# First chunk's products with u moved to GpSimd, loads reordered, and VectorE's bonus sum placed before the mask of its own step

## The chip, the cores and the metric

One core of one Trainium2 chip runs the whole program. The metric is the device time in microseconds of one execution, the median of several runs.

## The reference

Three layers in float32. First a linear attention over 4 batches, 8 heads, 768 tokens and 48 channels per head; its output, laid out as 3072 tokens of 384 numbers, goes through a soft mixture of experts (8 experts, 4 slots each) and then through a dense layer of width 2048 with a sigmoid gate. The change touches only the first layer:

```python
state = np.zeros((B, H, D, D), dtype=np.float32)
for t in range(S):
    kt, vt, rt = (k[:, :, t], v[:, :, t], r[:, :, t])
    cur = np.einsum('bhd,bhe->bhde', u[None] * kt, vt)
    y[:, :, t] = np.einsum('bhd,bhde->bhe', rt, state + cur)
    state = w[None, :, :, None] * state + np.einsum('bhd,bhe->bhde', kt, vt)
...
logits = x @ phi        # softmax over tokens and over slots, 8 experts: relu(slot @ w1) @ w2
...
h = x @ w_in
return (h * (1.0 / (1.0 + np.exp(-1.702 * h)))) @ w_out
```

The term with `u` is the "bonus": for each token and head, the sum over the 48 channels of r times k times u, times the token's v.

## The kernel before

The 768 tokens are cut into 6 chunks of 128, and in each chunk the 4 batches are done one after the other: 24 steps, numbered n = 4c + b for chunk c and batch b. Chunk 0 is written out, chunks 1 to 4 are a hardware loop, and chunk 5 is written out again. While the steps run, the weights of the expert layers are loaded beside the inputs of the steps. After step 23 come the expert layers and then the dense layer, in which TensorE does most of the work; nothing of that part is changed.

The order of the work is written out by hand for each engine, and semaphores tie the engines together. What one step consists of:

- **SyncE's queue** issues the loads of step n: `rk` (r and k with the channels on the partitions, 512 KB, tile `rkb`, two buffers), `kr` (k and r with the tokens on the partitions, 384 KB, tile `krb`, two buffers) and `v` (192 KB), and from chunk 1 on one or two 512 KB pieces of expert weights. The load of `rk` for step n waits until VectorE has scaled step n-2, and the load of `kr` for step n waits until GpSimd has made `kk` of step n-2.
- **VectorE** in step n: `scale` of step n+1 (L772, two operations, writes `rks`), which waits for the load and for `earlier` of step n-1 on TensorE (the last reader of the buffer); `mask` of step n (L798, two operations, copies the causal part of the scores into `at`); `bonus_sum` of step n+1 (L786, writes `dds`); `new_state` of step n-1 (L807). In a batch with b = 1 `slot_max` of the chunk before stands ahead of these, and with b = 3 `running` stands before `new_state`.
- **GpSimd** in step n: `bonus` (L1204, r times k into `rkn`, then L1209, times u, but in chunk 0 only the first of the two: there VectorE does the second at L782), `scaled_keys` (L1216, `kk`), `bonus_values` (L1226, writes `vd` from v and `dds`, so it waits for `bonus_sum` of step n). In the last chunk there are no `scaled_keys`; after the step with b = 1 eight small operations build `own` (L1245, L1246), after b = 2 the row maxima are subtracted (L1251), and in b = 3 the row factors are multiplied (L1240) before `bonus_values`.
- **TensorE** in step n: `earlier` of step n-1 (L414), `scores` of step n (L378), `outputs` of n-1 (L426), `state` of n-1 (L438), `tokens` of n-2 (L447), and from chunk 1 on, at the end of the step, `bonus_turns` of step n itself (L397), which reads `vd` of step n. In chunk 0 `bonus_turns` of the step before stands ahead of `outputs` instead, but for the last step of the chunk, which has both. `scores` wait for the masks of the step before and for `scale` of their own step.

Each engine takes its instructions in the order written, so an engine that waits holds all that stands behind the wait. In this text e is the time at which TensorE begins `earlier` in a step.

## Time and profile before

| | before |
|---|---|
| median of 3 runs | 385.12 us (384.98 to 385.4) |
| the profiled execution | 385.27 us, of which 383.5 us lie between its first and last instruction |
| TensorE busy | 369.9 us (96%), granted clock 1.00 throughout |
| VectorE, ScalarE, GpSimd busy | 235.0, 189.4, 94.5 us |
| data moved | 63.76 MB, nearly all in the first 160 us |

Busy time counts an engine's instructions, not its waits; for TensorE the ends of matmuls are modelled, so its share is high even where it is held up a little. The share is a mean over the whole span. What a change to the first layer is worth is read from the first 130 us: from the start of each instruction, and from what ended the idle time before it.

### The profile page before, as it was taken

To read this page: it belongs to the slowest core of one execution; us is meant where nothing else is said; L and a number is where in the kernel's file an instruction comes from. 1 tells how busy PE (TensorE), PEld (TensorE's weight loads), DVE (VectorE), ACT (ScalarE), POOL (GpSimd) and SP (SyncE) were. 2 spreads that over 40 slices of the span, in tenths; PEclk is the share of its full clock that TensorE was granted. 3 is DMA by queue.
4 is the path that set the end of the run, shared out by engine and by line. 5 is a ranking of instruction groups with operands and counts; after the bars stand their busy time and mean duration, and the time that the engine had idled before them with its cause. 6 is when DMAs were issued, how large, how long until landed. Compare 5 with 4: busy or idle time off the path is not lost.

```text
span 383.5 us, 9099 instructions
## 1 busy us (share of the span) xinstructions
PE 369.9 (96%) x3206; PEld 290.6 (76%) x3206; DVE 235.0 (61%) x433; ACT 189.4 (49%) x409; POOL 94.5 (25%) x110
## 2 busy tenths in 40 slices
PE   5698999999999999999999999999999999999996
PEld 5677788878777344577888888888888888888885
DVE  6978787878774301587756556555555555555550
ACT  1344554545434440676564456445644564465452
POOL 4678788878682020100000000000000000000000
PEclk9999999999999999999999999999999999999999
DMA  7899999999999999600011002000200020002002
GB/s 234 286 333 344 400 393 405 399 393 354 405 327 409 390 414 413 249 0 2 1 46 38 0 0 84 0 0 0 82 0 0 0 82 0 0 0 82 0 2 82
DMA packets 21797, 63.76 MB, mean 166 GB/s; under 512 B 3088, under 2 KB 6816, under 8 KB 21392
## 3 DMA queue, kind: packets, MB, share of 16 engines
q1 hardware_dynamic: 20864, 63.09, 43.4%
q10 hardware_dynamic: 912, 0.39, 0.5%
q8 instruction: 14, 0.23, 0.2%
q14 instruction: 7, 0.06, 0.0%
HBM read 58.75 MB, written 4.72 MB: 165 GB/s over the span
## 4 chain that ended last, share of the span: by engine, by line
PE 92%; DVE 2%; DMA 2%; issue 1%; ACT 1%; POOL 1%; SPq 0%; DVEq 0%; ACTq 0%
PE bank L638 11%; PE bank L637 11%; PE bank L636 11%; PE bank L378 6%; PE pair L426 6%; PE pair L636 6%; PE pair L637 6%; PE pair L638 6%; PE bank L623 4%; PE pair L414 3%; PE pair L397 3%; PE bank L585 3%; PE bank L447 3%; PE bank L565 2%; DMA vb<-v 2%; PE bank L438 2%
## 5 line engine op out<-in xcount | busy, mean ns | idle before, releaser
L926 DVE TENSOR_TENSOR gf<-bank,sg 128x512 f32<-128x512 f32 x72 | 49.8, 691 | 58.3 <-ACT sg L1133 58.0
L1133 ACT ACTIVATE sg<-bank 128x512 f32<-128x512 f32 x72 | 42.9, 598 | 71.0 <-PE bank L623 71.0
L637 PE MATMUL bank<-ghi,whi 128*128 128x512 f32 x190 | 73.9, 389 | 0.0
L636 PE MATMUL bank<-glo,whi 128*128 128x512 f32 x190 | 73.9, 389 | 0.0
L638 PE MATMUL bank<-ghi,wlo 128*128 128x512 f32 x190 | 73.9, 389 | 0.0
L937 DVE TENSOR_TENSOR glo<-gf,ghi 128x512 fp32r<-128x512 f32 x96 | 66.3, 691 | 0.3
L1139 ACT ACTIVATE ghi<-gf 128x512 fp32r<-128x512 f32 x95 | 59.3, 624 | 1.8 <-DVE gf L926 1.7
L636 PEld LDWEIGHTS bank<-glo,whi 128*128 128x128 f32 x190 | 35.7, 188 | 7.4
L637 PEld LDWEIGHTS bank<-ghi,whi 128*128 128x128 f32 x190 | 35.7, 188 | 7.4
L638 PEld LDWEIGHTS bank<-ghi,wlo 128*128 128x128 f32 x190 | 35.7, 188 | 7.4
L772 DVE TENSOR_TENSOR rks<-rkb,bank 112x512 f32<-112x512 f32 x48 | 30.8, 681 | 15.4 <-PE pair L414 10.9
L636 PE MATMUL pair<-glo,whi 128*128 128x512 f32 x95 | 37.3, 392 | 0.0
L637 PE MATMUL pair<-ghi,whi 128*128 128x512 f32 x95 | 37.0, 389 | 0.0
L638 PE MATMUL pair<-ghi,wlo 128*128 128x512 f32 x95 | 37.0, 389 | 0.0
L798 DVE COPY_PREDICATED at<-keep,bank 128x512 f32<-128x512 int32 x48 | 32.5, 730 | 1.3 <-PE bank L378 0.9
L378 PE MATMUL bank<-rks 48*128 48x128 f32 x384 | 27.9, 284 | 5.2 <-DVE rks L772 3.9
L926 DVE TENSOR_TENSOR gf<-pair,sg 128x512 f32<-128x512 f32 x24 | 16.6, 692 | 23.8 <-ACT sg L1133 23.7
L378 PEld LDWEIGHTS bank<-rks 48*128 48x128 f32 x384 | 23.4, 187 | 9.5 <-issue 8.0
L1016 ACT ACTIVATE yt<-pair 112x512 f32<-112x512 f32 x24 | 14.3, 598 | 30.0 <-PE pair L426 30.0
L623 PE MATMUL bank<-ct,mst 128*128 (+1 forms) x72 | 27.9, 392 | 0.5 <-DVE mst L964 0.4
L1204 POOL TENSOR_TENSOR rkn<-krb 128x384 f32<-128x384 f32 x24 | 24.1, 1004 | 12.2 <-DMA krb<-kr 11.9
L426 PE MATMUL pair<-at,vb 128*48 128x128 f32 x384 | 25.9, 277 | 0.0
(179 smaller groups left out, 512.3 us busy)
## 6 DMA issues: line engine op xcount, KB each, us to landing
ring<-w SPq DMA_DIRECT2D x24, 512.0 KB, 6.3
rkb<-rk SPq DMA_DIRECT2D x23, 512.0 KB, 6.2
krb<-kr SPq DMA_DIRECT2D x24, 384.0 KB, 5.5
ring<-w SPq DMA_DIRECT2D x4, 1536.0 KB, 14.3
ring<-w SPq DMA_DIRECT2D x8, 768.0 KB, 8.4
vb<-v SPq DMA_DIRECT2D x24, 192.0 KB, 5.5
out<-ob SPq DMA_DIRECT2D x18, 256.0 KB, 2.1
ring<-win SPq DMA_DIRECT2D x3, 1024.0 KB, 14.3
```

Of the source, the lines that this page charges most:

```text
L378: last = pe.matmul(SC[i][:, hp * CH:(hp + 1) * CH], rks[s, b % 2, 1, hp, :], rks[s, b % 2, 0, hp, :], start=True, stop=True)
L426: last = pe.matmul(YT[i][o0:o0 + D, a * CH:(a + 1) * CH], vb[:, b, 2 * (a + 2 * w) + i, :], at[:, b % 2, i, a + 2 * w, :], start=False, st ...
L623: pe.matmul(HB[f % 4][:, :], mst[:, f * P:(f + 1) * P], ct_flat[:, bass.ds(i * TT, TT)], start=True, stop=True).then_inc(hh_ps, 1)
L636: pe.matmul(o, w_hi, lo, start=(f == 0), stop=False)
L637: pe.matmul(o, w_hi, hi, start=False, stop=False)
L638: pe.matmul(o, w_lo, hi, start=False, stop=(f == KF - 1)).then_inc(prod_ps, 1)
L772: dve.tensor_tensor(rks[a, b % 2, x, :, :], rkb[a, b % 2, x, :, :], w[a, :, :], ALU.mult)\
L798: dve.copy_predicated(at[:, b % 2, half, :, :], keep[:, :].unsqueeze(1).to_broadcast([P, 4, CH]), SC[half][:, :].rearrange("p (h t) -> p h ...
L926: dve.tensor_tensor(gf[:, f % 2, :], bank[f % 4][:, :], sg[:, f % 2, :], ALU.mult).then_inc(gf_ok, 1)
L937: dve.tensor_tensor(glo[:, f % 4, :], gf[:, f % 2, :], ghi[:, f % 4, :], ALU.subtract)\
L1133: act.activation(sg[:, f % 2, :], bank[f % 4][:, :], ACT.Sigmoid, scale=1.702).then_inc(sg_ok, 1)
L1139: act.activation(ghi[:, f % 4, :], gf[:, f % 2, :], ACT.Copy).then_inc(ghi_ok, 1)
```

## The change

Eight edits. (1) In chunk 0 GpSimd multiplies by u itself (L1209 in all chunks) and VectorE's four operations at L782 are gone. (2) The load of u moves from ScalarE's queue to SyncE's, as its fourth load, behind `rk` and `kr` of step 0, with a semaphore of its own. (3) The loads of steps 2 and 3 stand in another order: rk2, v2, rk3, kr2, v3, kr3 in place of rk2, kr2, v2, rk3, kr3, v3. (4) VectorE's `bonus_sum` in step n is that of step n, not n+1, and stands behind `scale` of n+1 and ahead of `mask` of n. (5) In steps 1 to 3 `scale` of the next step stands ahead of `mask`, and in step 0 behind `mask` and `bonus_sum`. (6) ScalarE no longer decays the state in chunk 0, where it is zero, and the counts that VectorE waits for follow. (7) Ten opening matmuls on the identity become nine. (8) Seven such matmuls behind the first scores become six.

```diff
--- before.py
+++ after.py
@@ -40,7 +40,7 @@
 LOWEST = -3.0e38
 EPS = 1e-9
 LEAD = 3
-WARM = 10
+WARM = 9
 
 
 def wait(eng, sem, value):
@@ -190,6 +190,7 @@
             sem(n) for n in ("sc_ps", "masked", "yt_ps", "yt_ok", "st_ps", "sdec", "s_new", "yn_ps", "yn_ok"))
         lt_ps, l_ok, cm_ok, nm_ok, ex_ok, al_ok, tr_ps, tr_ok, p_ps, run_ok = (
             sem(n) for n in ("lt_ps", "l_ok", "cm_ok", "nm_ok", "ex_ok", "al_ok", "tr_ps", "tr_ok", "p_ps", "run_ok"))
+        s_u = sem("s_u")
         nm_new, l_new, mask_go, tiles_go = (sem(n) for n in ("nm_new", "l_new", "mask_go", "tiles_go"))
         spr_ok, bc_ps, nf_ok, fac_ok, lf_ok, ls_ps, samef_ok, rden_ok, si_ps, si_ok = (
             sem(n) for n in ("spr_ok", "bc_ps", "nf_ok", "fac_ok", "lf_ok", "ls_ps", "samef_ok", "rden_ok", "si_ps",
@@ -294,12 +295,17 @@
 
             load_rk(0, 0)
             load_kr(0, 0)
+            sp.dma_start(ubc[:, :, :].rearrange("p h e -> p (h e)"), u.partition_broadcast(P)).then_inc(s_u, 16)
             load_rk(0, 1)
             load_v(0, 0)
             load_kr(0, 1)
             load_v(0, 1)
-            step(0, 2, 0, 0)
-            step(0, 3, 0, 0)
+            load_rk(0, 2)
+            load_v(0, 2)
+            load_rk(0, 3)
+            load_kr(0, 2)
+            load_v(0, 3)
+            load_kr(0, 3)
 
             for dst, src in ((same[:, :], match), (jcol[:, :], jsel), (pick[:, :, :], sel)):
                 sp.dma_start(dst, src).then_inc(s_late, 16)
@@ -384,7 +390,7 @@
                     for i in range(HP):
                         last = pe.transpose(YN[:, i * P:i * P + PAIR], wks[0:PAIR, i, :], idt[0:PAIR, 0:PAIR])
                     last.then_inc(wkn_ps, 1)
-                    keep_warm(LG, 7)
+                    keep_warm(LG, 6)
 
             def bonus_turns(c, b):
 
@@ -774,13 +780,6 @@
 
             def bonus_sum(c, b):
                 n = B * c + b
-                if is_first(c):
-
-                    dve.wait_ge(rk_ok, n + 1)
-                    if b == 0:
-                        dve.wait_ge(s_const, 16 * 2)
-                    dve.tensor_tensor(rkn[:, b % 2, :, :], rkn[:, b % 2, :, :], ubc[:, :, :], ALU.mult)\
-                       .then_inc(rku_ok, 1)
                 dve.wait_ge(rku_ok, n + 1)
                 wait(dve, vd_ok, n - 1)
                 dve.tensor_reduce(dds[:, b % 2, :], rkn[:, b % 2, :, :], AX_X, ALU.add).then_inc(dd_ok, 1)
@@ -789,7 +788,7 @@
                 n = B * c + b
                 if is_first(c, b):
                     dve.wait_ge(zeroed, 5)
-                    dve.wait_ge(s_const, 16 * 2)
+                    dve.wait_ge(s_const, 16)
                 for half in range(2):
                     dve.wait_ge(sc_ps, 2 * n + half + 1)
                     wait(dve, yt_ps, n - 1)
@@ -803,7 +802,11 @@
             def new_state(c, b):
                 n = B * c + b
                 dve.wait_ge(st_ps, n + 1)
-                dve.wait_ge(sdec, HP * (n + 1))
+
+                if is_first(c):
+                    dve.wait_ge(s_new, 1)
+                else:
+                    dve.wait_ge(sdec, HP * (n - B + 2))
                 dve.tensor_tensor(st[a, b, :, :].rearrange("p h e -> p (h e)"),
                                   st[a, b, :, :].rearrange("p h e -> p (h e)"), ST[a, 0:HP * D], ALU.add)\
                    .then_inc(s_new, 1)
@@ -848,17 +851,17 @@
                 more = not (is_last(c) and b == B - 1)
                 if tail and b == 1:
                     slot_max(c - 1)
-                if is_first(c) and b:
+                if is_first(c, b):
                     mask(c, b)
+                    bonus_sum(c, b)
                     scale(*following(c, b))
                 else:
                     if more:
                         scale(*following(c, b))
+                    bonus_sum(c, b)
                     mask(c, b)
                 if is_last(c) and b == 2:
                     row_sum(*early)
-                if more:
-                    bonus_sum(*following(c, b))
                 if tail and b == 3:
                     running(c - 1)
                 if not is_first(c, b) and not is_last(prev(c, b)[0]):
@@ -869,7 +872,6 @@
             scale(0, 0)
             dve.tensor_tensor(wks[a, :, :], wk[a, :, :], pw[a, 7, :].unsqueeze(2).to_broadcast([PAIR, HP, CH]),
                               ALU.mult).then_inc(wks_done, 1)
-            bonus_sum(0, 0)
             steps(dve, step)
 
             def low_weights(which, t):
@@ -993,9 +995,7 @@
         @block.scalar
         def _(act):
             act.dma_start(idt[:, :], ident).then_inc(s_ident, 16)
-            for dst, src in ((ubc[:, :, :].rearrange("p h e -> p (h e)"), u.partition_broadcast(P)),
-                             (keep[:, :], strict)):
-                act.dma_start(dst, src).then_inc(s_const, 16)
+            act.dma_start(keep[:, :], strict).then_inc(s_const, 16)
 
             act.wait_ge(wkn_ps, 1)
             act.activation(wkn[:, :, :].rearrange("p (h i) e -> p h i e", h=HP), YN[:, :].rearrange("p (h i e) -> p h i e", h=HP, i=2)[:, :, :, 0:D],
@@ -1061,7 +1061,7 @@
                     scales(c - 1)
                     kept_logits(c - 1)
                 if not is_first(c, b):
-                    if not is_last(prev(c, b)[0]):
+                    if not is_first(prev(c, b)[0]) and not is_last(prev(c, b)[0]):
                         decay(*prev(c, b))
                     columns(*prev(c, b))
                     if tail and b == 1:
@@ -1203,9 +1203,9 @@
                 wait(pool, dd_ok, n - 1)
                 pool.tensor_tensor(rkn[:, s, :, :], krb[:, s, 0, :, :], krb[:, s, 1, :, :], ALU.mult)\
                     .then_inc(rk_ok, 1)
-                if is_first(c):
-                    return
                 pool.wait_ge(rk_ok, n + 1)
+                if is_first(c, b):
+                    pool.wait_ge(s_u, 16)
                 pool.tensor_tensor(rkn[:, s, :, :], rkn[:, s, :, :], ubc[:, :, :], ALU.mult).then_inc(rku_ok, 1)
 
             def scaled_keys(c, b):
```

VectorE's instructions of chunk 0 before, from behind `wks` to the end of step 1 and the start of step 2 (`rkn` is the product r times k, `dds` the bonus sum, `rks` the scaled r and k, `at` the mask's output, `st` the state):

```order
L782 TENSOR_TENSOR rkn<-rkn,ubc 128x384
L786 TENSOR_REDUCE dds<-rkn 128x8
L772 TENSOR_TENSOR rks<-rkb,bank 112x512 x2
L798 COPY_PREDICATED at<-keep,bank 128x512 x2
L782 TENSOR_TENSOR rkn<-rkn,ubc 128x384
L786 TENSOR_REDUCE dds<-rkn 128x8
L798 COPY_PREDICATED at<-keep,bank 128x512 x2
L772 TENSOR_TENSOR rks<-rkb,bank 112x512 x2
```

The same place of the changed program, where lines have moved by a few (L778 is `scale`, L785 `bonus_sum`, L797 `mask`, L810 `new_state`):

```order
L797 COPY_PREDICATED at<-keep,bank 128x512 x2
L785 TENSOR_REDUCE dds<-rkn 128x8
L778 TENSOR_TENSOR rks<-rkb,bank 112x512 x4
L785 TENSOR_REDUCE dds<-rkn 128x8
L797 COPY_PREDICATED at<-keep,bank 128x512 x2
L810 TENSOR_TENSOR st<-st,bank 112x192
```

The products with u are gone; the first bonus sum now stands behind the first mask; and four scalings, those of steps 1 and 2, stand together.

VectorE's first loop step (b = 0 of a chunk) before:

```order
L772 TENSOR_TENSOR rks<-rkb,bank 112x512 x2
L794 REGISTER_ALU
L49 REGISTER_ALU
L798 COPY_PREDICATED at<-keep,bank 128x512
L794 REGISTER_ALU
L798 COPY_PREDICATED at<-keep,bank 128x512
L784 REGISTER_ALU
L786 TENSOR_REDUCE dds<-rkn 128x8
```

and in the changed program:

```order
L778 TENSOR_TENSOR rks<-rkb,bank 112x512 x2
L783 REGISTER_ALU
L49 REGISTER_ALU
L785 TENSOR_REDUCE dds<-rkn 128x8
L793 REGISTER_ALU
L797 COPY_PREDICATED at<-keep,bank 128x512
L793 REGISTER_ALU
L797 COPY_PREDICATED at<-keep,bank 128x512
```

Within a step the sum has moved ahead of the mask; what the rows do not show is that it is the sum of step n, where before it was that of step n+1, so that counted in steps it comes almost a step later.

GpSimd's first instructions behind its memory sets in the changed program (before, the two rows of L1209 were not there):

```order
L1204 TENSOR_TENSOR rkn<-krb 128x384
L1209 TENSOR_TENSOR rkn<-rkn,ubc 128x384
L1226 TENSOR_TENSOR vd<-vb,dds 128x2x4x48
L1216 TENSOR_TENSOR kk<-krb,wkn 128x384
L1204 TENSOR_TENSOR rkn<-krb 128x384
L1209 TENSOR_TENSOR rkn<-rkn,ubc 128x384
L1216 TENSOR_TENSOR kk<-krb,wkn 128x384
L1226 TENSOR_TENSOR vd<-vb,dds 128x2x4x48
```

From the second step on GpSimd's round in chunk 0 is now the one of all other chunks: two products, `kk`, `vd`.

## Rows read from the trace of the kernel before

**Rows 1.** Waits of TensorE: total us, times, longest us.

```profile
PE bank L378 <- DVE rks L772: 3.9, 3, 1.8
```

**Rows 2.** Timeline of the opening: start us, us, then the instruction.

```profile
2.84 4.05 PE L365 MATMUL bank<-idt 128*128 128x128 f32 x20 [2.84 <-DMA idt<-ident]
...
6.77 1.29 DVE L772 TENSOR_TENSOR rks<-rkb,bank 112x512 f32<-112x512 f32 x2 [1.58 <-DMA rkb<-rk]
...
8.20 1.16 PE L378 MATMUL bank<-rks 48*128 48x128 f32 x16 [1.32 <-DVE rks L772]
9.13 0.56 DVE L782 TENSOR_TENSOR rkn<-rkn,ubc 128x384 f32<-128x384 f32 x1 [0.47 <-POOL rkn L1204]
...
13.06 1.00 POOL L1216 TENSOR_TENSOR kk<-krb,wkn 128x384 f32<-128x384 f32 x1
13.14 1.34 DVE L782 TENSOR_TENSOR rkn<-rkn,ubc 128x384 f32<-128x384 f32 x1 [0.42 <-POOL rkn L1204]
...
26.10 0.65 PE L414 MATMUL pair<-rks,st 48*48 48x128 f32 x16
```

**Rows 3.** Busy times in one stretch; last columns TensorE's clock, DMA share, GB/s.

```profile
2.80:6.90 4.10, 4.05 (x20) 3.86 (x20) 2.52 (x29) 0.66 (x1) 1.32 (x1) 1.00 0.83 229
```

**Rows 4.** Timeline of GpSimd: one `vd` and the next, a full round apart.

```profile
23.06 0.83 POOL L1226 TENSOR_TENSOR vd<-vb,dds 128x384 f32<-128x384 f32 x1 [1.22 <-DVE dds L786]
...
26.86 0.83 POOL L1226 TENSOR_TENSOR vd<-vb,dds 128x384 f32<-128x384 f32 x1
```

**Rows 5.** Timeline of an ordinary step, chunk 4, b = 2.

```profile
92.31 0.65 PE L414 MATMUL pair<-rks,st 48*48 48x128 f32 x16
...
93.10 1.28 DVE L772 TENSOR_TENSOR rks<-rkb,bank 112x512 f32<-112x512 f32 x2 [0.68 <-PE pair L414]
...
94.30 1.36 DVE L798 COPY_PREDICATED at<-keep,bank 128x512 f32<-128x512 int32 x2
...
95.56 0.53 DVE L786 TENSOR_REDUCE dds<-rkn 128x8 f32<-128x384 f32 x1
95.84 0.65 PE L397 MATMUL pair<-idt,vd 128*112 128x128 f32 x4
```

**Rows 6.** Timeline of steps with b = 0, in chunks 4 and 5.

```profile
82.96 0.65 PE L414 MATMUL pair<-rks,st 48*48 48x128 f32 x16
...
84.39 1.28 DVE L772 TENSOR_TENSOR rks<-rkb,bank 112x512 f32<-112x512 f32 x2 [0.23 <-issue]
...
101.30 0.65 PE L414 MATMUL pair<-rks,st 48*48 48x128 f32 x16
...
102.28 1.29 DVE L772 TENSOR_TENSOR rks<-rkb,bank 112x512 f32<-112x512 f32 x2
```

**Rows 7.** Timeline of the last chunk, b = 1 to 3.

```profile
106.11 0.18 POOL L1245 MEMSET own<- 128x96 f32 x1
...
107.17 1.28 DVE L772 TENSOR_TENSOR rks<-rkb,bank 112x512 f32<-112x512 f32 x2 [0.20 <-PE pair L414]
...
107.61 1.01 POOL L1204 TENSOR_TENSOR rkn<-krb 128x384 f32<-128x384 f32 x1
...
108.69 1.01 POOL L1209 TENSOR_TENSOR rkn<-rkn,ubc 128x384 f32<-128x384 f32 x1
...
113.68 0.73 ACT L1055 ACTIVATE lnat<-lnat 128x640 f32<-128x640 f32 x1
113.84 0.65 PE L397 MATMUL pair<-idt,vd 128*112 128x128 f32 x4 [0.17 <-ACT yt L1016]
114.44 0.82 DVE L821 TENSOR_REDUCE rm<-lnat 128x20 f32<-128x640 f32 x1 [0.41 <-ACT lnat L1055]
115.86 1.26 POOL L1240 TENSOR_TENSOR lnat<-lnat,rm 128x640 f32<-128x640 f32 x1 [1.37 <-DVE rm L825]
118.77 0.60 PE L397 MATMUL pair<-idt,vd 128*112 128x128 f32 x4
```

**Rows 8.** The tile `krb`: from a load's issue to its landing.

```profile
DMA to landing us min/median/max: 3.2/5.5/8.4
```

## The prediction

> **What bounds the kernel now.** I read the totals first: TensorE is busy 369.9 of 383.5 us, so time is lost or won where TensorE waits or is made to wait. Its list of waits comes next. The largest that the list shows is 3.9 us for the scaled r and k, three times [rows 1]; with the 2.8 us until the identity has landed [rows 2] it falls into the opening. From 26.10 on TensorE runs from one instruction into the next. So there are two places to look at: the opening, where the change can win, and the 20 steps behind it, where it can only lose.
>
> In the opening TensorE's scores begin when the first `rk` has landed and been scaled: VectorE starts at 6.77, TensorE at 8.20, and `earlier` of the first loop step, the end of the opening for TensorE, starts at 26.10 [rows 2].
>
> An ordinary step shows how tight the rest is [rows 5]. TensorE begins at e = 92.31. VectorE's `scale` starts at e + 0.79, since it waits for `earlier`; its second half ends 1.20 later, where `mask` starts. `bonus_turns`, which reads `vd`, starts at e + 3.53 and waits for nothing, as its `vd` was made a step ahead: the sum that stands at 95.56 is that of the next step.
>
> **The change part by part.** Its own time before is 385.27 us (a span of 383.5 and 1.77 around it); the median of 385.12 lies 0.15 below, so I take 0.15 off at the end.
>
> *Opening.* u is 192 KB, and its load ran beside the first `rk`, in a stretch in which 229 GB/s were moved [rows 3]. 192 KB by that rate is 0.86 us, so with u behind it the first `rk` should land 0.86 earlier and `scale` start at 5.9 in place of 6.77. Scores begin 1.43 behind it, as now, and take 1.16: they end at 8.5. The first mask (1.36 [rows 5], about 0.1 behind the scores) ends at 9.95 and the first sum (0.53) at 10.5, and GpSimd starts `vd` of step 0. Its round then sets the pace: from one `vd` to the next it takes 3.80 with both products in it [rows 4], as it now has in chunk 0. `vd` and `kk` of step 0 take 0.78 and 0.97 to the next start, so the products of step 1 begin at 12.3, those of step 3 two rounds later at 19.9, and `vd` of step 3 starts 3.02 behind them and ends at 23.75. TensorE takes it up 0.1 later, turns it in 0.57, and begins `earlier` at 24.4 in place of 26.10: **-1.7**. VectorE must fit into this round: scale 1.20, sum 0.53 and mask 1.36 are 3.1, with a short state update less than 3.80. Bounds: if the first `rk` lands no earlier, -0.85; if u cost it twice its share, -2.6.
>
> The second product on VectorE took 1.34 where the first took 0.56 [rows 2]: it began beside a `kk` of GpSimd (13.06 to 14.06) and ended 0.42 after it. With the products on GpSimd this wait is gone, which is inside the sum above, since GpSimd's round sets the pace there. The Trainium skill (SBUF — State Buffer, section "SBUF: two separate sides") says that VectorE and GpSimd share one port pair under an exclusive lock: a vector instruction with two SBUF inputs is held for the whole of a GpSimd instruction that reads SBUF. By that rule the trace agrees with 1.34.
>
> u's load, now the third in SyncE's queue, delays the loads behind it by 0.86; GpSimd needs u only for a product at about 7.5, whose sum waits behind a mask until 9.95, so it costs nothing. Cover gone, it would cost its 0.86, as in the lower bound. The order of loads of steps 2 and 3 brings `rk` 3 ahead of `kr` 2; both are asked for (12.3) more than 3 us before GpSimd reads `kr` 2 (16.1), so I take nothing. The decays that are dropped run on ScalarE, which waits for TensorE anyway: nothing. The nine opening matmuls take 0.20 a pass (20 passes in 4.05 [rows 2]) and end at 6.5, before the scores at 7.3: nothing.
>
> *The 19 or so steps behind it.* `vd` of a step is now made within the step. From the start of `scale`: 1.20, sum 0.53, 0.08 to GpSimd, `vd` 0.83, and about 0.1 to TensorE, in all 2.75. In an ordinary step that is e + 0.79 + 2.75 = e + 3.54, and `bonus_turns` is due at e + 3.53 [rows 5]. So most of a step of slack is used up to the last tenth. I take 0.03 for each of 14 such steps, **+0.4**; bounds 0 and 0.1 each, 1.5.
>
> With b = 0 it is later, because VectorE comes out of `running` and `new_state` behind TensorE: `scale` starts at e + 1.43 in chunk 4 (84.39 against 82.96) and at e + 0.98 in chunk 5 (102.28 against 101.30) [rows 6]. The same instructions stand ahead of it in the changed order, only sum and mask have changed places. `vd` is then ready at e + 4.18 and e + 3.73, that is 0.65 and 0.2 late; less 0.05 for what the step before was held, about 0.6 in each of the chunks 2 to 4 and 0.2 in chunk 5: **+2.0**. TensorE has nothing behind to make up for it. Bounds: 0.2 in each of four, 0.8, and 0.75 in each, 3.0.
>
> *Last chunk.* GpSimd has the `own` tiles to build (106.11 to 107.61, 1.50) between `vd` of step b = 1 and the products of b = 2 (107.61 to 109.70, 2.09) [rows 7]. Now `vd` of b = 1 cannot start before 107.17 + 1.20 + 0.53 + 0.08 = 108.98. Then `own` from 109.76, products 111.26 to 113.35, sum to 113.9, `vd` to 114.8, TensorE at 114.9 in place of 113.84: 1.05 late. Behind that `vd` stands the subtraction (1.26, as long as the multiplication at 115.86) to 116.0, the exponential (0.73) to 116.8, row sum to reciprocal (114.44 to 115.86, 1.42) to 118.2, the multiplication to 119.5, `vd` of b = 3 to 120.35, TensorE at 120.45 in place of 118.77: **+1.7** in all. Bounds: the first wait alone, less the 0.17 it covers, 0.9; and 2.2 if the first load of `kr` in it is late too.
>
> Sum: -1.7 + 0.4 + 2.0 + 1.7 = +2.4, 387.65 for a profiled execution, **387.5** as a median.
>
> **The rivals.**
>
> *Faster.* The mechanism is that `vd` comes in time with b = 0 too: `scale` starts at e + 0.8 to 0.98 in all chunks, and in the last chunk only the first wait remains. Then -1.7 + 0 + 0.8 + 0.9 is 0.0, and with an opening of -2.6 it is -0.9: 384.3. For it speaks that chunk 5 shows e + 0.98; against it that the loop's round shows 1.43, and that the turn to the next round lies in it. It decides at the point where all waits of TensorE for `vd` together are less than what the opening gives. 0.17, at 384.3.
>
> *Cancelled.* Opening and waits are of one size, as the 0.0 just worked out: 385.1. 0.12.
>
> *The loads starve.* `vd` of a step now ends at e + 3.44; two products (2.1) and a `kk` (1.0) behind it, at about e + 6.5, `kr` of three steps on from e is asked for, and it is due when GpSimd wants it, 3.1 ahead of its own `vd` at e + 2.6 of that step. That leaves three steps of 4.1 to 4.9 less 6.5 and 0.5, some 6.1 to 7.1 us, where a landing takes 5.5 and at most 8.4 [rows 8]. If landings stay as spread as now, half of the 20 steps could be held by 0.3: +3, 390.5. Against it speaks that requests which come later find a shorter queue. 0.07.
>
> *VectorE is held by GpSimd.* At the chunk's turn VectorE's small two-input operations fall beside GpSimd's products. The hold seen is 0.42 behind the start of a product [rows 2]; if the start of `scale` with b = 0 came later by twice that in each of the three loop rounds, it would be +2.5: 390.0. By the skill's rule named above a hold may last a whole GpSimd instruction, which has the same effect. 0.06.
>
> **How the numbers follow.** Forecast 0.58, faster 0.17, cancelled 0.12, starved 0.07, held 0.06. The likeliest case gives 387.5; its own range, with its terms moved inside their bounds, is 386.1 to 389.3. To hold eight in ten the range goes from 384.5, which leaves out about half of the faster case, to 389.6, which leaves out the two slow rivals: 0.1 and 0.1. About 0.2% (0.77 us) is what a measurement of this kernel can tell from no change. Slower by over that: 0.58 + 0.07 + 0.06 = 0.71; within: 0.12; faster: 0.17.
>
> **What the changed profile would show.** `scale` of step 0 starts near 5.9, and `earlier` of the first loop step near 24.4. The waits of TensorE hold a new line, `bonus_turns` for `vd`, with some 4 us in total: about 0.6 in each b = 0 step of the loop, one of about 1 and one of over 0.5 in the last chunk, near nothing elsewhere. GpSimd in turn waits for `dds` in nearly every step. From the end of the last step on everything stands at one distance to before. I am wrong if the line sums to less than 2 us, or if the opening gives over 3, or if GpSimd waits for `kr` and TensorE behind it.

## The result: 12 us slower, four fifths of it unforeseen

| | before | changed |
|---|---|---|
| median | 385.24 us (383.87 to 387.06, 6 runs) | 397.49 us (395.33 to 400.68, 6 runs) |
| the profiled execution | 385.27, span 383.5 | 398.65, span 396.9 |

The ratio is 1.032 (95% interval 1.027 to 1.037). The forecast of 387.5 (384.5 to 389.6) had the sign right and the size wrong by 10 us.

The page of the changed kernel: the span, TensorE's busy time, and the strips of TensorE's granted clock and of the DMA engines' share, each sign a fortieth of the span.

```profile
span 396.9 us, 9072 instructions
PE 375.5 (95%) x3202; PEld 293.6 (74%) x3202; DVE 234.7 (59%) x429; ACT 186.0 (47%) x397; POOL 97.8 (25%) x114
PEclk9996999999999999999999999999999999999999
DMA  6899889999999979940002000200100020002002
```

Its waits: total us, times, longest us. SPq is SyncE's queue.

```profile
DVE rks L778 <- DMA rkb<-rk: 10.7, 5, 3.1
PE pair L403 <- POOL vd L1226: 9.9, 11, 2.0
POOL rkn L1204 <- DMA krb<-kr: 2.4, 2, 1.9
SPq L278 <- POOL kk L1216: 47.4, 20, 4.0
```

The queue's wait for `kk` in the kernel before, and its wait for VectorE's `scale`, before and then changed:

```profile
SPq L277 <- POOL kk L1216: 27.3, 18, 3.7
SPq L269 <- DVE rks L772: 19.0, 17, 3.9
SPq L270 <- DVE rks L778: 7.5, 5, 4.8
```

The first row of TensorE's wait list before was 3.9 us for the scaled r and k [rows 1]. Now `bonus_turns` (L403) waits 9.9 us for `vd`, where the forecast said some 4. Two other rows were not in the forecast at all: VectorE's `scale` waits 10.7 us for the load of `rk` (3.8 before), and SyncE's queue waits 47.4 us for `kk` before it can ask for `kr`. Part of that wait has only moved: before, the queue stood as long for either, 27.3 us for `kk` and 19.0 for `scale`; now it is 47.4 and 7.5, so that the sum rose from 46.3 to 54.9. GpSimd itself hardly waits for `kr` (2.4 us).

The starts of `earlier` locate the loss. The first is at 25.88 (26.10 before [rows 2]), the last at 132.68 (119.30 before). That difference, 13.4 us, is the whole difference of the spans, so nothing behind the chunks matters. By steps (from one `earlier` to the next, worked out from the timelines; the last row is a run that comes below, e13):

```
chunks 2, 3, 4, 5     b=0                     b=1                     b=2                     b=3
before                5.12 5.11 5.11 5.05     4.24 4.24 4.24 4.03     4.89 4.89 4.89 4.82     4.15 4.20 4.10 4.10
changed               6.03 6.18 6.11 5.82     4.57 4.57 4.57 4.18     4.88 4.89 4.88 5.79     4.95 5.63 5.09 4.96
e13                   6.04 6.14 6.13 5.80     4.57 4.57 4.56 4.18     4.88 4.89 4.89 5.79     4.15 4.15 4.11 4.95
chunk 1: before 5.11 5.85 4.88 4.18; changed 7.39 7.15 4.89 4.27; e13 5.31 4.56 4.89 4.26
```

One figure of the kernel before is not an ordinary step: in the second step of chunk 1 (5.85 where the later chunks take 4.24) TensorE stood for 1.20 us behind the first twelve matmuls of `earlier`, with nothing in the trace that it waited for:

```profile
33.05 0.42 PE L414 MATMUL pair<-rks,st 48*48 48x128 f32 x4 [1.20 <-issue]
```

The same step takes 5.33 to 5.68 in e2, e8, e10 and e12 and 4.24 in e6 and e14, below; no run shows what it is. The changed kernel has no such row.

So of 13.4: opening -0.2; b = 0 +3.75; b = 1 +1.15; the last chunk's b = 2 and 3 +1.8; b = 3 in chunks 2 to 4 +3.2; chunk 1 +3.7.

A step with b = 3 in the changed kernel (chunk 3), which ends at 91.28 with the next `earlier`:

```profile
76.55 1.00 POOL L1216 TENSOR_TENSOR kk<-krb,wkn 128x384 f32<-128x384 f32 x1
77.71 0.33 SPq L278 DMA_DIRECT2D krb<-kr  x1
80.54 0.33 SPq L270 DMA_DIRECT2D rkb<-rk  x1
...
85.65 0.65 PE L420 MATMUL pair<-rks,st 48*48 48x128 f32 x16
...
87.92 1.28 DVE L778 TENSOR_TENSOR rks<-rkb,bank 112x512 f32<-112x512 f32 x2 [3.12 <-DMA rkb<-rk]
89.12 0.55 DVE L785 TENSOR_REDUCE dds<-rkn 128x8 f32<-128x384 f32 x1
89.74 0.83 POOL L1226 TENSOR_TENSOR vd<-vb,dds 128x384 f32<-128x384 f32 x1 [2.53 <-DVE dds L785]
90.63 0.65 PE L403 MATMUL pair<-idt,vd 128*112 128x128 f32 x4 [1.33 <-POOL vd L1226]
```

Read it from the end. TensorE waits for `vd`, `vd` for the sum, and the sum stands on VectorE behind a `scale` that has waited 3.12 us for `rk`. The loads of `rk` around here landed 6.4 to 7.2 us after they were asked for, so the one that ends this wait is that of 80.54. It was asked for so late because it stands in the queue behind `kr` of the step before, two pieces of w (only steps with b = 3 load two) and v; that `kr` had waited for `kk`, which ended at 77.55. And `kk` stands on GpSimd behind `vd`. The circle is closed: a late `vd` makes the next `kk`, `kr` and `rk` late, and with them a later `vd`. It starts at the steps with b = 0, where `vd` is late by the sum's place in the order.

### The profile page after: what moved, and what is told of

Its sections match the earlier page's. It is cut to its first block, busy times and chain, and to the rows that moved or that the text cites. A ratio compares the mean times of both kernels' runs of the same rounds, so it can differ in the third digit from the quotient of the medians.

```text
span 396.9 us, 9072 instructions
## 1 busy us (share of the span) xinstructions
PE 375.5 (95%) x3202; PEld 293.6 (74%) x3202; DVE 234.7 (59%) x429; ACT 186.0 (47%) x397; POOL 97.8 (25%) x114
## 4 chain that ended last, share of the span: by engine, by line
PE 73%; POOL 9%; issue 6%; DMA 5%; DVE 4%; SPq 1%; DVEq 1%; ACT 0%; POOLq 0%; ACTq 0%
PE bank L642 11%; PE bank L643 11%; PE bank L644 11%; PE pair L642 6%; PE pair L643 5%; PE pair L644 5%; PE bank L629 4%; DMA rkb<-rk 3%; PE bank L591 3%; PE bank L384 2%; POOL vd L1226 2%; POOL rkn L1209 2%; POOL rkn L1204 2%; PE bank L571 2%; POOL kk L1216 2%
## 5 line engine op out<-in xcount | busy, mean ns | idle before, releaser
L778 DVE TENSOR_TENSOR rks<-rkb,bank 112x512 f32<-112x512 f32 x48 | 30.8, 682 | 20.8 <-DMA rkb<-rk 10.7
L797 DVE COPY_PREDICATED at<-keep,bank 128x512 f32<-128x512 int32 x48 | 32.2, 725 | 2.5 <-PE bank L384 2.5
L384 PE MATMUL bank<-rks 48*128 48x128 f32 x384 | 29.7, 297 | 3.6 <-DVE at L797 2.1
L384 PEld LDWEIGHTS bank<-rks 48*128 48x128 f32 x384 | 24.9, 199 | 8.2 <-issue 5.7
L928 DVE TENSOR_TENSOR gf<-pair,sg 128x512 f32<-128x512 f32 x24 | 16.6, 691 | 23.1 <-ACT sg L1133 22.9
L1226 POOL TENSOR_TENSOR vd<-vb,dds 128x384 f32<-128x384 f32 x24 | 19.9, 830 | 31.4 <-DVE dds L785 31.4
L432 PE MATMUL pair<-at,vb 128*48 128x128 f32 x384 | 26.8, 283 | 0.0
```

The costliest lines, as they stand in the source:

```text
L384: last = pe.matmul(SC[i][:, hp * CH:(hp + 1) * CH], rks[s, b % 2, 1, hp, :], rks[s, b % 2, 0, hp, :], start=True, stop=True)
L778: dve.tensor_tensor(rks[a, b % 2, x, :, :], rkb[a, b % 2, x, :, :], w[a, :, :], ALU.mult)\
L797: dve.copy_predicated(at[:, b % 2, half, :, :], keep[:, :].unsqueeze(1).to_broadcast([P, 4, CH]), SC[half][:, :].rearrange("p (h t) -> p h ...
L928: dve.tensor_tensor(gf[:, f % 2, :], bank[f % 4][:, :], sg[:, f % 2, :], ALU.mult).then_inc(gf_ok, 1)
L1226: pool.tensor_tensor(vd[:, b % 2, :, :, 0:D].rearrange("p x w e -> p w x e"), vb[:, b, :, :].rearrange("p (w x) e -> p w x e", w=2), dds[: ...
```

## The experiments

Theory A: the loss is the new order on VectorE from chunk 1 on. Theory C: most of it comes by way of the loads, as in the circle above, and not from `vd`'s own lateness. Rivals: the opening's edits do harm, the granted clock, GpSimd's queue. In each job the kernel before ran beside the others: medians 384.49 (e1 to e4), 384.94 (e5 to e8), 385.24 (e9 to e12) and 385.66 us (e13 to e15).

**e1: the kernel before with edit 4 alone, from chunk 1 on.**

```diff
                     if more:
                         scale(*following(c, b))
+                    if tail:
+                        bonus_sum(c, b)
                     mask(c, b)
...
-                if more:
+                if is_first(c) and b < B - 1:
                     bonus_sum(*following(c, b))
```

> The kernel before, with one edit: from chunk 1 on VectorE's bonus sum is that of its own step and stands ahead of the mask. Theory A (VectorE's order alone makes the kernel slow, directly and through loads that are asked for later): 394 to 398 us, TensorE waits for vd by 7 to 10 us in all, VectorE waits for rkb by 8 us or more. Rival B (the opening's edits put the loads behind, and they never catch up): 386 to 389 us, with only the waits that were forecast.

Measured: 396.41 us (394.64 to 398.57), ratio 1.032. The order alone gives the whole loss, and the same rows (L397 for `vd` 8.9 us, `scale` for `rk` 12.5, the queue for `kk` 43.9).

**e2: the changed kernel with the old order from chunk 1 on**, the inverse of that diff.

> The changed kernel with VectorE's order of before from chunk 1 on; the opening stays changed. Theory A: 384 to 386 us, TensorE does not wait for vd behind chunk 0. Rival B: 390 us or more, VectorE still waits for rkb by over 8 us. If the opening gives what was forecast for it (1.7), 383.5.

Measured: 385.15 us (384.22 to 386.28), ratio 1.002 (1.0003 to 1.0037). Its waits, in the fastest of its ten runs (384.22), the one that was profiled:

```profile
DVE rks L778 <- DMA rkb<-rk: 5.3, 5, 1.6
SPq L278 <- POOL kk L1219: 29.0, 20, 2.2
```

So the other seven edits together bring nothing, though `earlier` of the first loop step stood at 25.17 here: what the opening gained was no gain in the time.

**e3: the changed kernel with `rk` asked for a step ahead**, in front of `kr` in the queue.

```diff
             def step(c, b, first, count):
-                load_rk(c, b)
+                if not (is_last(c) and b == B - 1):
+                    load_rk(*following(c, b))
                 load_kr(c, b)
```

> The changed kernel, where from chunk 1 on SyncE asks for rk one step ahead, in front of the kr load that waits for GpSimd's kk. Theory C (rk is late because it stands behind that wait in the queue): VectorE's waits for rkb fall from 10.7 us to under 3, TensorE's waits of 0.7 to 2.0 us in the steps with b = 3 and in the first loop step go, the clock does not fall: 388.5 to 391.5 us. Rival D (rk is late because the transfers themselves are slow or the buffer is freed late): 396 us or more. The waits in b = 0 (0.6 to 0.95 each) and in the last chunk stay under both.

Measured: 390.27 us (388.11 to 391.59), ratio 1.0135. `scale` waits for `rk` 3.3 us in place of 10.7 (under 3 was expected), TensorE for `vd` 7.2:

```profile
POOL rkn L1206 <- DMA krb<-kr: 14.1, 15, 1.8
PE pair L405 <- POOL vd L1228: 7.2, 9, 1.5
DVE rks L780 <- DMA rkb<-rk: 3.3, 2, 2.2
SPq L278 <- POOL kk L1218: 5.9, 6, 2.2
```

7.2 of the 12.3 us are gone (6.5 against the kernel before of its own job) with one load moved in one queue, while VectorE's order is untouched.

**e4: the changed kernel with eight dummy matmuls ahead of `bonus_turns` in the loop's steps with b = 0**, to keep TensorE busy while it waits.

> The changed kernel with eight matmuls on the identity in the loop steps with b = 0, ahead of the instruction that waits for vd; they fill 0.9 us of a wait of 0.8 to 2.0. Theory E (the granted clock fell to half from 33 to 40 us because TensorE had stood idle for 2 us just before): the clock stays at 1.00, the stretch from the first loop step to the third takes about 11 us in place of 14.5, 393 to 395 us. Rival F (the fall has another cause): the clock falls as before, 397 us or more.

Measured: 396.62 us (395.40 to 398.15), a miss in the time. The granted clock did not fall in chunk 1, but it fell in the last chunk, behind a wait that the dummies do not fill (timeline, then the granted clock, DMA share and GB/s at the end of each window):

```profile
123.63 0.62 PE L403 MATMUL pair<-idt,vd 128*112 128x128 f32 x4 [1.99 <-POOL vd L1229]
...
126.00:128.00 2.00, 2.00 (x28) 1.64 (x22) 1.43 (x4) 0.31 (x1) 1.58 (x2) 0.50 1.02 418
```

The dummies were not free either: the b = 0 steps of chunks 2 to 4 took 6.83 where the changed kernel took 6.03 to 6.18. So the run shows that a busy TensorE kept its clock in chunk 1, and not what that is worth.

**e5: edits 7 and 8 undone in the changed kernel; e8: the same in e2.**

```diff
-WARM = 9
+WARM = 10
...
-                    keep_warm(LG, 6)
+                    keep_warm(LG, 7)
```

> The changed kernel with the opening's twenty dummy products and the longer run of matmuls ahead of the first scores put back. If the opening loses its gain because TensorE meets the first scores at the lower clock, scores(0, 0) takes about 1.16 us in place of 2.08 and the first step's products come up to 0.9 us earlier: 396.6 to 397.1 us, against 397.5 for the changed kernel. If the opening is set by what VectorE and the loads of rk do behind the first scores, the 20 passes buy nothing: 397.3 to 397.8. Neither expects more than 1 us, and the spread of this kernel's runs (395.3 to 400.7) may hide it in the time; the profile's rows of the opening decide.

> The kernel with the old order of VectorE from chunk 1 on and the changed opening (385.15 us), with the twenty dummy products and the longer run ahead of the first scores put back. If the changed opening's gain is lost to the lower clock under the first scores: 384.0 to 384.6 us. If it is lost behind them: 384.9 to 385.4, the same.

Measured: e5 396.75 us (395.28 to 397.70), e8 385.06 us (384.10 to 386.45), ratio 1.0002 (0.9988 to 1.0015). No gain: the first scores now began at 7.40 in place of 6.92 and took 1.43 us in e5 and 1.91 in e8, so that they ended at 8.83 and 9.31; in the changed kernel it was 9.00. Of the two times only e8's can tell: four runs of e5 spread over 2.4 us.

**e6: from chunk 1 on the sum stands ahead of `scale`.**

```diff
+                    if tail:
+                        bonus_sum(c, b)
                     if more:
                         scale(*following(c, b))
-                    bonus_sum(c, b)
+                    if not tail:
+                        bonus_sum(c, b)
                     mask(c, b)
```

> The changed kernel, but from chunk 1 on bonus_sum of a step stands ahead of the next step's scale on VectorE, so that GpSimd's bonus product no longer stands behind a scale that waits for rk. If the coupling through scale is what costs (sum late because scale waits for rk, rk late because kr stands behind GpSimd's kk, kk late because the product waits for the sum), the loop is cut: TensorE's waits for the product go to under 3 us in all and the time comes to 385 to 388 us. If the sum stays late by its own place (behind new_state and mask) or the scale, pushed back, now holds the scores, it stays at 393 us or above.

Measured: 386.11 us (385.43 to 387.12), ratio 1.0022 (1.0005 to 1.0038). Its waits:

```profile
DVE rks L778 <- DMA rkb<-rk: 12.1, 8, 2.3
PE pair L403 <- POOL vd L1229: 1.7, 4, 0.9
```

This is the plainest of the runs. The sum is still that of its own step, as in the change, and VectorE still waits 12.1 us for `rk`; but the sum no longer stands behind that wait, and 11.4 of the 12.3 us of the changed kernel are gone (11.1 against the kernel before of its own job).

**e7: e3 with the last chunk's `own` tiles built ahead of `vd`.**

> The kernel in which rk is asked for a step ahead of kr (390.3 us), and in which GpSimd builds the last chunk's own tiles ahead of the bonus product, in the time in which it waits for the sum. If the last chunk's wait (1.16 us in that kernel) is GpSimd's queue, it goes: 389.0 to 389.6 us. If the product is late there by the sum, building the tiles first changes nothing or puts the product later: 390.3 to 391.

Measured: 390.84 us (387.96 to 393.30), no gain in the time where 0.7 to 1.3 us was expected: a miss, in runs that spread over 5 us. At its place the wait fell from 1.16 to 0.62 us and the step from 5.79 to 5.24; so GpSimd's queue was half of that wait.

**e9, e10, e11: `rk` a step ahead, as in e3, in e2, in e6 and in the kernel before.**

> The kernel with the old order of VectorE from chunk 1 on and the changed opening (385.15 us), with rk asked for a step ahead of kr. Its only wait of TensorE for the bonus product is 0.80 us in chunk 0, behind a scale that waits 1.46 us for rk. If that wait is the place of rk in SyncE's queue, it goes and the time comes to 384.0 to 384.6 us. If the opening's gain is lost elsewhere (the lower clock under the first scores, kr then being the late load), the time stays at 384.9 to 385.5.

> The kernel in which the sum stands ahead of the next scale (386.1 us), with rk asked for a step ahead. If what is left of its loss is scale waiting for rk: 385.0 to 385.6 us. If it is the 0.16 to 0.28 us waits for the product, which come from the sum's own place in the step: 386.1 as before, within 0.4. It also shows that both cures of one loop don't add up: either alone takes away 7.2 and 11.4 of the 12.2 us.

> A control: the kernel before, with only rk asked for a step ahead of kr. In the kernel before VectorE waits 3.8 us for rk, off TensorE's path behind the opening. So no change in the time: 384.5 to 385.2 us, the measured median of the kernel before within 0.3. If it comes out faster by over 1 us, the gain of the run with rk ahead is a gain of any order, and says nothing on the loop.

Measured: e9 402.11 us (400.29 to 403.39), e10 395.79 (391.65 to 397.52), e11 405.36 (404.76 to 407.68), ratio 1.052. All three missed, and by much: what had brought 7 us in e3 costs 10 to 20 in the other orders. The waits of e11:

```profile
POOL rkn L1206 <- DMA krb<-kr: 38.5, 20, 4.0
DVE dds L788 <- POOL rkn L1211: 27.5, 17, 4.4
SPq L269 <- DVE rks L774: 63.0, 20, 5.6
```

With `rk` ahead, `kr` now stands behind a load that waits for `scale` (63.0 us). In the changed kernel's order that is affordable. In the old one GpSimd's products are wanted a step earlier, so `kr` is the load without slack. That is read from these waits, and no run tests it by itself. The e3 result holds for the changed order only.

**e12: e2 with ScalarE copying `yt` three times in step b = 0 and five times in step b = 2 of the last chunk** (the same data), a wait of known length for TensorE.

> The kernel with the old order and the changed opening (385.15 us), in which ScalarE copies yt three times in place of once in step b = 0 of the last chunk, and five times in step b = 2; the data are the same. TensorE should idle about 1.2 us ahead of one bonus_turns and about 2.5 us ahead of the other. If a wait costs only itself: 388.6 to 389.2 us and a granted clock of 1.00 throughout. If the clock falls behind a wait of some 2 us of TensorE, as behind 1.99 us in the changed kernel, and not behind one of 1.2: a stretch of 0.50 to 0.55 for some 6 us behind the second wait, none behind the first, and 391.5 to 393 us.

Measured: 389.31 us (388.69 to 391.57). The waits and the windows behind them:

```profile
109.96 0.65 PE L403 MATMUL pair<-idt,vd 128*112 128x128 f32 x4 [1.21 <-ACT yt L1020]
...
112.00:120.00 8.00, 6.93 (x94) 4.88 (x90) 5.65 (x13) 3.49 (x6) 4.47 (x5) 1.00 1.02 414
...
121.33 0.76 PE L403 MATMUL pair<-idt,vd 128*112 128x128 f32 x4 [2.24 <-ACT yt L1020]
...
122.00:124.00 2.00, 2.00 (x27) 1.61 (x28) 0.69 (x1) 0.15 (x1) 0.00 (x0) 0.50 1.03 421
```

Behind 1.21 us the clock stays at 1.00, behind 2.24 it falls, as expected, but for some 3 us and not 6: from `earlier` to the logits it took 4.01 us where e2 took 2.60, so the fall cost 1.4. The time, 389.31, came out near the 388.6 to 389.2 of the rival and under the 391.5 to 393 expected with a fall.

**e13, e14, e15: the 24 loads of w moved behind all loads of the chunks**, in the changed kernel, in the one before and in e11. The expert layers then wait for w (414.9, 409.5 and 422.0 us in all), so the last `earlier` is read.

```diff
                 load_v(c, b)
-                load_w1(first, count)
...
                 step(C - 1, b, (B + 1) * (C - 2) + b, 1)
+            load_w1(0, (B + 1) * (C - 2) + B)
```

> The changed kernel, with the 24 loads of w (512 KB each, 5 of the 17 loads of a chunk) moved behind all loads of the chunks, so that the DMA engines have 4352 KB to move in a chunk in place of 6912. The feed-forward part behind the chunks then waits for w, so the reading is the start of the last earlier, 132.68 in the changed kernel and 119.30 in the one before. If a late kk turns into a late rk because the DMA engines are full (their share in the loop is 0.99 to 1.04 before, and a gap in the requests is never made up): TensorE's waits for the product fall to the forecast 4 us and less, and the last earlier comes at 120 to 124. If it is SyncE's order alone, whatever the engines have to move: 129 or later.

> The control: the kernel before with the same 24 loads moved. Its TensorE waits for nothing in the loop, so the last earlier stays at 119.3, within 0.5, by either theory; only VectorE's 3.8 us of waits for rk and GpSimd's for kr shrink.

> The kernel before with rk asked for a step ahead of kr (405.4 us, last earlier at 141.62, GpSimd waits 38.5 us for kr), with the same 24 loads moved. If the full DMA engines are what makes kr late: kr lands some 2 us sooner, GpSimd's wait falls under 10 us and the last earlier comes at 119 to 124. If the place in the queue alone does it: 130 or later.

Measured, last `earlier`: e13 124.75 (132.68 with w in the loop), e14 118.97 (119.30), e15 131.07 (141.62). e13 stands 0.75 outside the 120 to 124 expected, far from the 129 of the other case. e14 agrees in sum, but by two differences that cancel: its first `earlier` came 1.31 us later than in the kernel before, at 27.41, and the 1.20 us stand of chunk 1 is not there. The waits of e13:

```profile
PE pair L403 <- POOL vd L1226: 4.5, 6, 1.2
DVE rks L778 <- DMA rkb<-rk: 2.3, 2, 1.9
SPq L278 <- POOL kk L1216: 54.9, 20, 4.0
```

The stretch from 45 to 120, in the kernel before, the changed one and e13 (last three columns as above):

```profile
45.00:120.00 75.00, 74.81 (x1306) 60.85 (x1304) 60.19 (x121) 36.79 (x112) 59.11 (x69) 1.00 1.02 385
```

```profile
45.00:120.00 75.00, 68.43 (x1216) 55.15 (x1210) 55.57 (x107) 33.39 (x107) 52.47 (x56) 1.00 0.94 338
```

```profile
45.00:120.00 75.00, 70.16 (x1224) 56.20 (x1228) 57.43 (x109) 33.11 (x106) 55.64 (x67) 1.00 0.73 247
```

The queue waits as long as ever for `kk` (54.9 us), but the median landing of `rk` is 4.8 us in place of 6.5, and the circle does not close: the b = 3 steps in the table are back at 4.15. So with w away 7.9 of the 13.4 us are gone (6.3, if each kernel is read from its first to its last `earlier` and e13 is set against e14). In the kernel before the engines were full (share 1.02, 385 GB/s); in the changed one the share is 0.94 at TensorE's later pace.

But e13 does two things at once. The pieces of w are gone from the engines, and from SyncE's queue too, where they stood between `kr` and the next `rk`. The same two loads in e13, in the chunk of the rows above:

```profile
72.24 0.33 SPq L278 DMA_DIRECT2D krb<-kr  x1
...
73.66 0.33 SPq L270 DMA_DIRECT2D rkb<-rk  x1
```

From `kr` to `rk` it takes 1.42 us here and 2.83 with two pieces of w between them (77.71 to 80.54), so `rk` is asked for 1.41 sooner; the landing takes 4.7 us here in the median of this stretch and 6.5 there. With b = 3 VectorE wanted `rk` 0.80 behind the start of `earlier` in e13 (80.99 against 80.19), and in the changed kernel it came 2.27 behind (87.92 against 85.65), 1.47 too late. As an estimate from these rows, either of the two alone would about have done: asked for at 79.13 and landing in 7.2 us, `rk` comes at 86.3, asked for at 80.54 and landing in 4.7 us at 85.2, and it was wanted at 86.45. How much full engines cost by themselves is thus not shown.

Theory C was right for half of the loss: 6.9 of the 13.4 us lie in chunk 1 and the b = 3 steps of chunks 2 to 4, where `rk` is late, and 6.7 in the steps with b = 0, b = 1 and the end of the last chunk, which keep their loss in e13 and are late by the sum's own place.

In e15 half of e11's loss (10.6 of 22.3) stays away. 131.07 lies in the range of the case in which the place in the queue alone does it (130 or later), and GpSimd still waits 26.1 us for `kr`, where under 10 was expected if full engines made it late.

## Why the prediction was wrong

By its own steps:

- *What bounds the kernel.* "From 26.10 on TensorE runs from one instruction into the next" (but for the 1.20 us at 33.05), so the sum has VectorE's `scale` start when TensorE lets it, at e + 0.79 and e + 1.43, and no term for a load. **This is the step that failed.** In the b = 3 step above `scale` started at e + 2.27, behind 3.12 us of waiting for `rk`; in all that wait grew from 3.8 to 10.7 us, and the sum now stood behind it. e6, with the sum ahead of `scale`, is nearly free of the loss though VectorE waits 12.1 us. The places without a term, b = 3 in chunks 2 to 4 (+3.2) and chunk 1 (+3.7), hold 6.9 of the 11.0 us between the forecast +2.4 and the measured +13.4; the opening holds 1.5, b = 0 1.75, the ordinary steps 0.7, the last chunk 0.1. I had quoted a GB/s for the opening only [rows 3], and did not see that the engines stood at 1.02 in the steps behind it; e14 shows that in the kernel before this cost nothing: from chunk 2 on its steps without w are the same to 0.02 us.
- *Opening, -1.7.* It gave -0.2 in the profile and nothing in the time (e2). That -0.2 is one draw: with this same opening the first `earlier` stands at 24.79 to 25.93 (e2, e4, e6, e12, e13), with the old one at 25.98 to 27.41 (e1, e14). `scale` began at 5.17, sooner than the 5.9 expected, but the scores took 2.08 us and not 1.16, so the products of step 1 began at 12.84 (forecast 12.3). The dummy passes, which I had end at 6.5 and cost nothing, took 4.21 us to 6.99, and the scores followed at 6.92 without a wait; with twenty of them (e5, e8) they began at 7.40. Two waits followed for which I had taken nothing:

```profile
12.91 0.33 SPq L278 DMA_DIRECT2D krb<-kr  x1
...
17.25 1.01 POOL L1204 TENSOR_TENSOR rkn<-krb 128x384 f32<-128x384 f32 x1 [0.58 <-DMA krb<-kr]
...
22.53 1.29 DVE L778 TENSOR_TENSOR rks<-rkb,bank 112x512 f32<-112x512 f32 x2 [1.12 <-DMA rkb<-rk]
24.36 0.83 POOL L1226 TENSOR_TENSOR vd<-vb,dds 128x384 f32<-128x384 f32 x1 [0.27 <-DVE dds L785]
25.33 0.62 PE L403 MATMUL pair<-idt,vd 128*112 128x128 f32 x4 [0.46 <-POOL vd L1226]
```

  `kr` of step 2, which edit 3 puts behind `rk` of step 3, took 4.3 us to land where I had said that 3 would do, and `rk` of the loop's first step came at 22.5. `vd` of step 3 began at 24.36 in place of 22.9.
- *No term: the first loop steps, +3.7.* The second `rk` of the loop landed when it had before (`scale` at 28.66, before at 28.56), but now `vd` hangs on it, and TensorE waits 1.99 us. Behind this wait the clock fell, and the second step took 7.15 us where it takes 4.56 in e13, 2.6 more (against the kernel before, with its stand of 1.20 us in that step, 1.3 more):

```profile
31.52 0.65 PE L403 MATMUL pair<-idt,vd 128*112 128x128 f32 x4 [1.99 <-POOL vd L1226]
...
34.00:36.00 2.00, 2.00 (x24) 1.70 (x16) 1.96 (x4) 1.49 (x8) 0.46 (x1) 0.50 0.90 352
```

- *Ordinary steps, +0.4.* With b = 2 they kept their time to 0.01, as forecast (4.89). With b = 1 they lost 0.33 each, 1.15 in all: `scale` starts at e + 1.29 in chunk 4 where it was e + 1.11, behind a `slot_max` that ends later (see the hold below), and the sum is on the path.
- *Steps with b = 0, +2.0.* Measured +3.75, above the bound of 3.0; the waits themselves are 0.80, 0.91, 0.89 and 0.59 in e13, where 0.6, 0.6, 0.6 and 0.2 were forecast. The mechanism was right and the size too small. In chunk 4 of e13:

```profile
84.34 0.65 PE L420 MATMUL pair<-rks,st 48*48 48x128 f32 x16
...
86.02 1.28 DVE L778 TENSOR_TENSOR rks<-rkb,bank 112x512 f32<-112x512 f32 x2 [0.23 <-issue]
...
88.88 0.65 PE L403 MATMUL pair<-idt,vd 128*112 128x128 f32 x4 [0.89 <-POOL vd L1226]
```

  `scale` starts at e + 1.68, not at e + 1.43 [rows 6]: "the same instructions stand ahead of it" was true, but one of them, the small update of the running sum (128x1, L838 before, L841 now), ends later. Before, and then in e13, with GpSimd's instruction beside it:

```profile
81.97 1.00 POOL L1216 TENSOR_TENSOR kk<-krb,wkn 128x384 f32<-128x384 f32 x1 [0.48 <-PE bank L438]
82.52 0.47 DVE L838 SCALAR_TENSOR_TENSOR stat<-stat 128x1 f32<-128x1 f32 x1
...
83.60 1.00 POOL L1204 TENSOR_TENSOR rkn<-krb 128x384 f32<-128x384 f32 x1
83.95 0.67 DVE L841 SCALAR_TENSOR_TENSOR stat<-stat 128x1 f32<-128x1 f32 x1
```

  In both it ends 0.02 behind GpSimd's instruction: 82.99 against 82.97, 84.62 against 84.60. GpSimd's instruction stands later in the step in e13, since the `vd` ahead of it had waited 1.07 us for the sum. The second operation of `slot_max` (L831, L834) does the same in the b = 1 steps, 0.90 us in chunks 2 to 4 of e13 and 0.01 to 0.02 behind the end of `kk`; with nothing of GpSimd beside them the two take 0.21 us (before, at 118.44) and 0.16 us (e13, at 110.29). The Trainium skill (SBUF — State Buffer, section "SBUF: two separate sides") describes such a hold between a vector instruction with two SBUF inputs and a GpSimd instruction that reads SBUF, in which whichever of the two engines starts first keeps the shared ports for its whole instruction; the trace agrees, with ends that follow GpSimd's by 0.02 us. The rival "VectorE is held by GpSimd" was thus real, at 0.25 a step. It had taken 0.42 for the hold of rows 2, where the second product took 0.78 longer than the first (1.34 against 0.56).
- *Last chunk, +1.7.* Measured +1.8: 0.97 and 0.86 in the two steps. Right, and the first wait is the one described: 1.17 us for `vd`, forecast 1.05.
- *The rival "the loads starve", 0.07.* Its kind was right and its load wrong. I followed `kk` to `kr` and `kr` to GpSimd, which indeed waits only 2.4 us, and stopped; behind that `kr` in the same queue stood `rk`. "Requests which come later find a shorter queue" held for `kr`, of which it was said (median landing 5.5 us before, 4.8 now), and not for `rk` (6.2 and 6.5).
- *What would show it wrong.* None of its three signs came: the line has 9.9 us, not under 2, the opening gave 0.2, and GpSimd hardly waits for `kr`. It had no sign for a line far over the 4 us that it gave, nor for a wait for `rk`.

Not settled: how the 7.9 us that go away in e13 divide between full engines, the place of w in the queue and the clock. The clock took 2.6 of them in the profiled execution, but e1 lost most of the time without it: its profiled run, 395.42 us, stood at 1.00 throughout.

## What to carry to other kernels

Before moving an operation to a later place in a step, follow the buffers that it frees through the DMA queue: every load behind the one that waits is late too. Put a sum that another engine waits for ahead of an operation that waits for a load, not behind it (e6). And an order of loads is good or bad only for one order of use: the same move gave 7 us in one kernel and took 20 in the other.

## What was unexpected of the hardware

The DMA engines moved 385 GB/s over 75 us in the kernel before, and 418 in stretches of e4. The Trainium skill (DMA: Bandwidth & Descriptors, section "Specifications") gives 435 GB/s as the ceiling of the fabric and about 358 for a core's share of HBM; here, with one core at work, the rows lie above the second and below the first.
